# Linear attention and two mixtures of experts in one kernel: a unit's outputs placed beside the next unit's state products

## The reference

```
def _attn_ref(q, k, v, f_logit):
    f = 1.0 / (1.0 + np.exp(-f_logit))
    for t in range(S):
        state = f[:, :, t, :, None] * state + np.einsum('bhd,bhe->bhde', k[:, :, t], v[:, :, t])
        y[:, :, t] = np.einsum('bhd,bhde->bhe', q[:, :, t], state)

def _moe_ref(x, domain_probs, w1, w2):
    p = domain_probs / (domain_probs.sum(-1, keepdims=True) + 1e-09)
    for e in range(E):
        out += p[:, e:e + 1] * (np.maximum(x @ w1[e], 0.0) @ w2[e])
```

## Time and profile before

| | us |
|---|---|
| median of 3 runs (1073.31 to 1074.09) | 1073.92 |
| the profiled execution | 1075.53 |
| its span in the trace | 1073.8 |
| TensorE busy in the span | 1029.2 |
| units 5 to 31 with the first expert's pieces, about | 56.5 to 345 |

### The profile page before, as it was taken

How to read it: one execution, slowest core, us unless ns; L and a number is a source line. 1 busy time by engine, 2 the same in 40 slices (tenths; PEclk the granted TensorE clock), 3 DMA queues, 4 the chain that set the end, 5 groups by cost and what they waited for, 6 DMA issues and landing times.

```text
span 1073.8 us, 17708 instructions
## 1 busy us (share of the span) xinstructions
PE 1029.2 (96%) x6997; PEld 966.1 (90%) x6997; DVE 358.6 (33%) x773; ACT 279.9 (26%) x577; POOL 88.4 (8%) x109
## 2 busy tenths in 40 slices
PE   5799999999999999999999999999999999999895
PEld 5688888888899899999999999999999999999543
DVE  4545454554644222222222222222222222222323
ACT  3343233232332331111114111111322222222322
POOL 1340100001000230000005000000220000000000
PEclk9699999999999999999999999999999999999897
DMA  9522343323420330000000300000030004020684
GB/s 218 115 61 57 73 80 66 61 57 75 83 56 13 124 118 1 0 0 0 0 1 1 117 0 0 0 0 0 0 118 1 1 1 176 0 79 1 240 328 176
DMA packets 129761, 67.04 MB, mean 62 GB/s; under 512 B 106656, under 2 KB 125088, under 8 KB 129696
## 3 DMA queue, kind: packets, MB, share of 16 engines
q1 hardware_dynamic: 129696, 66.18, 22.3%
HBM read 56.72 MB, written 4.72 MB: 57 GB/s over the span
## 4 chain that ended last, share of the span: by engine, by line
PE 93%; DVE 2%; SPq 2%; issue 1%; DMA 0%; ACT 0%; DVEq 0%; ACTq 0%
PE ph L1242 13%; PE po L1261 12%; PE po L1259 12%; PE ph L1244 12%; PE po L1260 12%; PE ph L1243 12%; PE pair L1194 2%; PE pc L1218 2%; PE pair L1162 2%; PE pc L1223 2%; PE pair L1174 1%; PE ph L1391 1%; PE po L1406 1%; PE pair L1164 1%; PE pc L1202 1%
## 5 line engine op out<-in xcount | busy, mean ns | idle before, releaser
L969 DVE SCALAR_TENSOR_TENSOR h_lo<-ph,h_hi 128x384 fp32r<-128x384 f32 x256 | 142.6, 557 | 503.4 <-ACT h_hi L736 502.7
L736 ACT ACTIVATE h_hi<-ph 128x384 fp32r<-128x384 f32 x256 | 126.0, 492 | 563.6 <-PE ph L1244 563.6
L1242 PE MATMUL ph<-xT,w_hi 128*128 128x384 f32 (+1 forms) x768 | 266.4, 347 | 2.2 <-DVE xT L950 2.2
L1259 PE MATMUL po<-w_hi,h_hi 128*128 128x384 f32 x768 | 259.3, 338 | 0.0
L1244 PE MATMUL ph<-xT,w_lo 128*128 128x384 f32 (+1 forms) x768 | 257.3, 335 | 0.0
L1261 PE MATMUL po<-w_hi,h_lo 128*128 128x384 f32 x768 | 257.1, 335 | 0.0
L1243 PE MATMUL ph<-xT,w_hi 128*128 128x384 f32 (+1 forms) x768 | 256.9, 335 | 0.0
L1260 PE MATMUL po<-w_lo,h_hi 128*128 128x384 f32 x768 | 256.7, 334 | 0.0
L1242 PEld LDWEIGHTS ph<-xT,w_hi 128*128 128x128 f32 x768 | 144.2, 188 | 8.8 <-issue 4.7
L1243 PEld LDWEIGHTS ph<-xT,w_hi 128*128 128x128 f32 x768 | 144.4, 188 | 0.0
L1259 PEld LDWEIGHTS po<-w_hi,h_hi 128*128 128x128 f32 x768 | 144.2, 188 | 0.2
(11 more groups left out here) (169 smaller groups left out, 711.2 us busy)
## 6 DMA issues: line engine op xcount, KB each, us to landing
v<-in_moe_w_dram SPq DMA_DIRECT2D x15, 1536.0 KB, 10.7
raw<-in_moe_w_dram SPq DMA_DIRECT2D x8, 1536.0 KB, 8.8
f_in<-in_f_logit_dram SPq DMA_DIRECT2D x48, 96.0 KB, 2.6
k_in<-in_k_dram SPq DMA_DIRECT2D x48, 96.0 KB, 2.6
q_in<-in_q_dram SPq DMA_DIRECT2D x48, 96.0 KB, 2.6
v_in<-in_v_dram SPq DMA_DIRECT2D x48, 96.0 KB, 2.6
out_dram<-out_sb SPq DMA_DIRECT2D x5, 768.0 KB, 5.5
x_raw<-yT SPq DMA_DIRECT2D x48, 72.0 KB, 2.2
```

The source lines that it names most:

```text
L736: a.activation(h_hi[:, f % 2, :], ph[f % 2][:, 0:BLK], ACT.Relu).then_inc(h_hi_done, 1)
L969: d.scalar_tensor_tensor(out=h_lo[:, f % 2, :], in0=ph[f % 2][:, 0:BLK], scalar=0.0, in1=h_hi[:, f % 2, :].bitcast(F32), op0=ALU.max, op1= ...
L1242: t.matmul(bank, wh, xh, start=(kk == 0), stop=False, skip_group_check=True)
L1259: t.matmul(bank, hh, w2_hi[:, f, :], start=(f == 0), stop=False, skip_group_check=True)
```

## The change

There are four parts.

1. The products of a unit become a step of their own, `P`, after `S`. They go into spare columns of the same pair banks as the scores (384 to 479 of the first bank, 384 to 431 of the second). DVE now waits for the products before it masks, and in the same place for the outputs of the unit before.
2. `Y` of unit u moves behind `P` of unit u + 1, except for the last unit of a half (u % 4 == 3), whose Y keeps its place two pieces after P.
3. The running sums of C and D go to `pc` in place of `pair`, and C or D moves behind the unit's fourth piece, so that it stands directly ahead of the next unit's T.
4. Waits follow: C and D wait for the copied outputs and for the sums before them, Y for the sums taken from `pc`, T for the state additions of the unit before. `qT` alternates between two tiles.

```diff
@@ first_stage
         steps.append(("S", u, None))
+        steps.append(("P", u, None))
+        if u > LAG and u % PER_HALF:
+            steps.append(("Y", u - 1, None))
...
         steps.append(pieces[n + 2])
-        steps.append(("Y", u, None))
+        if u % PER_HALF == PER_HALF - 1:
+            steps.append(("Y", u, None))
+        steps.append(pieces[n + 3])
         if m + 1 < UNITS // 2:
             steps.append(("D" if u % 2 else "C", m + 1, None))
-        steps.append(pieces[n + 3])
...
+        def products_of(u, c):
+
+            at_col = BLK + (c if c < BT - 1 else 0) * D
+            return pair_of(u)[:, 0 if c < BT - 1 else 1, at_col:at_col + D]
+
         def sums_bank(m, part):
-            return ph[part] if m <= 2 else bT
+            return ph[part] if m <= 2 else bST
+
+        def before_y(u):
+
+            return 0 if u < LAG else min(u + (2 if u % PER_HALF == PER_HALF - 1 else 3), 2 * QUADS)
...
             def scores(u):
...
-                dve.wait_ge(s_filled, u + 1)
+                dve.wait_ge(p_filled, u + 1)
+                at_least(dve, y_filled, before(u) + 1)
...
-                dve.wait_ge(p_filled, u + 1)
-                bank = last_of(u)
...
-                        new = bank[rows, c * D:(c + 1) * D]
+                        new = products_of(u, c)[rows, :]
...
                 if m <= 2:
                     at_least(pe, c_taken, 2 * (m - 1) + part + 1)
                 else:
-                    pe.wait_ge(s_masked, 2 * (m - 1) + part + 1)
+                    u = 2 * (m - 1) + part
+                    pe.wait_ge(y_taken, u + 1 if u < LAG or u % PER_HALF == PER_HALF - 1 else u)
+                    pe.wait_ge(c_taken, 2 * m + part)
...
                 at_least(pe, s_masked, before(u) + 1)
+                at_least(pe, st_done, st_count(before(u) + 1))
...
-                if m >= 2:
-                    pe.wait_ge(c_taken, 2 * m + i + 2 if m + 1 < QUADS else 2 * QUADS)
...
-                mm.then_inc(s_filled, 1)
-                bank = last_of(u)
-                at_least(pe, y_taken, before(u) + 1)
+
+            def products(u):
+                m, i = divmod(u, 2)
                 pe.wait_ge(v_landed[m % 2], loaded(m))
...
                 pe.wait_ge(s_masked, u + 1)
                 pe.wait_ge(st_done, st_count(u + 1))
+                at_least(pe, y_taken, before(u) + 1)
+                at_least(pe, c_taken, before_y(u))
```

More of the change, by code:

```diff
@@ L27 @@
 OPENING = (
-    "G0 L0 C0 D0 G1 L1 T0 T1 C1 D1 S0 S1 Y0 Y1 T2 T3 G2 L2 S2 S3 C2 D2 Y2 Y3 "
-    "W0 W1 T4 G3 S4 L3 X0 W2 Y4 C3"
+    "G0 L0 C0 D0 G1 L1 T0 T1 C1 D1 S0 P0 S1 P1 Y0 Y1 T2 T3 G2 L2 S2 P2 S3 P3 C2 D2 Y2 Y3 "
+    "W0 W1 T4 G3 S4 P4 L3 X0 W2 Y4 C3"
 )
@@ L186, in build @@
     kT = [small("kT0", [P, BLK]), small_at(second, "kT1", [P, BLK])]
-    qT = [small("qT0", [P, BLK]), small_at(second, "qT1", [P, BLK])]
+    qT = [small(f"qT{i}", [P, BLK]) for i in range(2)]
     masked = [small("masked0", [P, 2, BT, P]), small_at(second, "masked1", [P, 2, BT, P])]
@@ L281, in build @@
         qT_done = sem("qT_done")
-        s_filled = sem("s_filled")
         p_filled = sem("p_filled")
@@ L701, in turn @@
                 act.wait_ge(q_turned, u + 1)
-                a.activation(qT[set_of(u)][:], pair_of(u)[:, 1, 0:BLK], ACT.Copy).then_inc(qT_done, 1)
+                a.activation(qT[u % 2][:], pair_of(u)[:, 1, 0:BLK], ACT.Copy).then_inc(qT_done, 1)
             def outputs(u):
@@ L1193, in scores @@
                         rows = slice(WIN * hh, WIN * (hh + 1))
-                        mm = t.matmul(banks[:, hh, cols], kT[s][rows, cols], qT[s][rows, cols], start=True, stop=True)
-                mm.then_inc(s_filled, 1)
-                bank = last_of(u)
-                at_least(pe, y_taken, before(u) + 1)
+                        mm = t.matmul(banks[:, hh, cols], kT[s][rows, cols], qT[u % 2][rows, cols], start=True, stop=True)
+            def products(u):
+                m, i = divmod(u, 2)
                 pe.wait_ge(v_landed[m % 2], loaded(m))
@@ L1201, in scores @@
                         head = 2 * i + hh
-                        mm = t.matmul(bank[WIN * hh:WIN * (hh + 1), c * D:(c + 1) * D], kd[m % 2][:, c, head, :],
+                        mm = t.matmul(products_of(u, c)[WIN * hh:WIN * (hh + 1), :], kd[m % 2][:, c, head, :],
                                       v_in[m % 2][:, c, head * D:(head + 1) * D], start=True, stop=True)
@@ L1222, in outputs @@
                             state = st[s][:, c - 1, hh, :] if c else carry[:, r, hh, :]
-                            mm = t.matmul(bank[WIN * hh:WIN * hh + D, cols], state, qT[s][:, cols],
+                            mm = t.matmul(bank[WIN * hh:WIN * hh + D, cols], state, qT[u % 2][:, cols],
                                           start=False, stop=True, skip_group_check=True)
@@ L1253, in sums @@
                     pe.wait_ge(y_taken, 4)
+                    pe.wait_ge(st_done, st_count(4))
                 if f == 0:
@@ L1273, in _ @@
                     scores(i)
+                elif kind == "P":
+                    products(i)
                 elif kind == "Y":
```

## The result

The changed kernel takes 1136.31 us (median of 4 runs, 1135.97 to 1136.37) against 1074.01 before: 1.0577 times as long, 95% interval 1.0563 to 1.0590. That is 62.3 us more. The forecast was 1128, with a range of 1102 to 1150.

A forecast was written before the change was run, and what follows sets the result against it. PE was taken to bound units 5 to 31, busy 284.30 of 288.50 us. The terms 20.3 + 20.4 + 3 - 4 + 2.2 + 12 = 53.9 on 1073.92 gave 1128 us, range 1102 to 1150.

The forecast's parts named there:

- Part 1: T directly behind D in odd units: the 2.83 us chain uncovered, 1.56 us at each of 13 places, +20.3 us.
- Part 2: k and q loaded late for C's multiplies, so S waits about 3.4 us at six places: +20.4 us.
- Part 3: DVE's queue at the units with X (8, 12, ... 28): C's multiplies enter the gap, 0.5 us each, +3 us.
- Part 4: Y joined to P and C to T: two fewer small/large matmul edges in about 20 units, -4 us.
- Part 5: Opening: C of quad 3 waits for unit 4's copied outputs, and DVE masks later; +2.2 us, from 0 to 4.
- Part 6: TensorE's clock falls behind 7 of 19 gaps, 1.7 us lost each: +12 us, from 0 to 32.
- the likeliest case: Both waits come and the clock falls at some gaps: 1128 us, 1120 to 1138, chance 0.5.
- The rival of full clock: Both waits come in units 5 to 31 but the clock stays up: 1116 us, chance 0.2.
- the one with loads in time: k and q arrive in time for C's multiplies, so Part 2 and its falls go: 1100 us, chance 0.12.
- The rival in which nearly every gap pays: The clock falls at nearly every gap ahead of T and S: 1148 us, chance 0.13.

The follow-up runs named there:

- filled gaps: Changed kernel with PE's idle time ahead of T of even units and S of units 7, 11, ... 27 filled by matmuls whose result is overwritten: 1113.8 us.
- the outputs in their place: Changed kernel, but Y of every unit stands two pieces behind its own S and P, as before the change: 1100.0 us.
- the first four edits: Edits of the changed kernel: C and D ahead of the fourth piece (1115.4 us), loads ahead of stores (1102.4), both (1076.6), idle time filled with matmuls (1113.8).
- the early loads: Changed kernel, but for units 5, 9, ... 25 SP issues gate, k and q loads ahead of the wait for the unit's copied outputs: 1102.4 us.
- the sums a piece earlier: Changed kernel, but C and D stand ahead of the unit's fourth piece again, so a piece lies between D and T: 1115.4 us.

## Why the prediction was right, point by point

The terms are set against units 5 to 31, from the starts of PE's instructions. The kernel with filled gaps serves as the changed kernel without the clock.

| part | forecast | measured |
|---|---|---|
| 1, T behind D | +20.3 | +21.2 |
| 2, late k and q | +20.4 | +23.6 |
| 3, DVE's queue at X | +3 | +0.4 |
| 4, joined edges | -4 | -7.8 |
| 5, opening | +2.2 | -0.3 |
| 6, clock | +12 | +24.2 |

**Part 1** held as it was worked out. The idle time at T is 25.3 us, and 4.1 of it were there before, so 21.2 are new. The number of places (13) and the chain's length (2.83, then 2.79) were both read rightly, and moving D back took T's waits away.

**Part 2** had the right place, number and cause. Each of the six costs 3.9 us rather than 3.4. In the one shown, the loads of k took 2.18 us on SP and not 1.54 as before; what held them the profile does not say.

**Part 3** was too high. With the loads late, X did not become the last to finish; the six S concerned start 0.42 us after the piece ahead, before 0.35.

**Part 4** was undersized by half. I counted two edges of 0.1 us; the rows of the changed kernel at P of unit 13 and Y of unit 12 show where the rest was:

```profile
164.34 0.44 PE L1215 MATMUL pair<-v_in,kd 128*64 128x48 f32 x8
164.60 0.39 PE L1233 MATMUL pc<-masked,v_in 128*48 128x128 f32 x4
164.82 0.39 PE L1238 MATMUL pc<-qT,carry 128*48 128x128 f32 x4
```

P to Y is 0.26 us, where P to the piece h was 0.37; and where two blocks of small matmuls become one, a slow first step of h and a way into Y go as well. I put that at 0.38 us a unit in 19 units, an estimate. The measured figure is a remainder of the account, 288.3 + 21.2 + 23.6 + 0.4 - 325.7 = 7.8, so it holds whatever else the order changed; the estimate from the outputs in their place (7 us, above) agrees.

**Part 5** did not show in this kernel. The wait was there, 1.9 us ahead of C of quad 3. What gave as much back was the clock: the long low stretch of the opening ends at 51.1 us here and at 53.5 before. C and the T behind it, from the start of C to the first full piece, take 2.0 us instead of 4.2. C and the piece in the changed kernel, then the piece before:

```profile
52.38 0.59 PE L1176 MATMUL pc<-f_in,causal 128*128 128x192 f32 x2 [1.88 <-ACT yT L721]
54.35 0.42 PE L1257 MATMUL ph<-xT,w_hi 128*128 128x384 f32 x1
```

```profile
54.70 0.42 PE L1242 MATMUL ph<-xT,w_hi 128*128 128x384 f32 x1
```

The forecast of the opening had no term for the clock. With its low stretch the opening varies more than the term: S of unit 5 starts between 56.2 and 59.7 us in the five profiles of kernels that have the changed opening and differ only later (the changed kernel and the first four edits), and at 55.5 to 56.5 in three with the old one. The low stretch is 13.7 us long in two of the five, where S starts at 56.2, and 17.1 or 20.5 in the others; it is 13.7 in the three. So what the change itself costs there stays open.

**Part 6** was the largest miss, half of its value: 24.2 us instead of 12. I had taken 7 falls of 3.4 us each. The trace of the changed kernel has 11 low stretches in the units with 58 us in all. Which gaps bring it down was read rightly, few of the 13 and most of the six: it was five of the 13, 3.4 us each, and all six, 6.8 us each. Both the number and the length were too low. The length was taken from one low stretch near the end of the kernel, though the opening, where it also fell, has longer ones (6.8 us from 22.7 us on, 13.7 from 39.8). Half of 58 us would be 29; that 24.2 were lost fits low time that lies in the gaps, as the first microsecond of the stretch from 191 does. By number of falls the forecast lay between its two rivals.

So the likeliest case came true, 8 us low, and the misses of parts 3 to 5 (-9) hid part of those of 2 and 6 (+15). The rival of full clock (1116) was refuted by 20 us, the one with loads in time (1100) by 36. The rival in which nearly every gap pays (1148) was 12 us off, and the eight gaps of T without a fall speak against it. The Trainium skill ("TensorE: Matmul & The Clock Gate", HAM oscillation) describes a loop that is granted the low clock anew in every round, and its waits there are longer than the 13 gaps of 2 us here. The trace agrees with it for the six long gaps, and for five of the 13 short ones.

## What to carry to other kernels

Count the distance from an instruction to the one that needs its result in time, not in steps: a step that looked free to move was the whole cover of a 2.8 us chain. When a result is moved later, read what is queued behind the wait for it on every queue; here twelve loads on SP held X up for 3 us, and passing the finished half on before them gave 5 us (1072.3 to 1066.9) to a kernel without the change. And price a gap with its clock: here 50 us of waits brought 24 us more.

## What had not been expected of the hardware

**Equal gaps, unequal clock.** Gaps of 2 us ahead of T, with the same work next to them, had a fall behind 5 of 13 in the changed kernel, 8 of 13 with the early loads and 1 of 13 with the outputs back, in one profile of each. The last two had PE busy for 288 and 286 us in the units. The gaps of 3.2 to 5.4 us ahead of S had one each time, six of six in the changed kernel and six of six with the sums a piece earlier. So the length of a gap of 2 us alone does not decide it. What else does, perhaps when it comes, was not tried.

**The clock at the end.** The part after the units is the same program in all of these kernels, and in the profiled executions took 727.5 to 734.0 us. The longest had the low clock for 30 us of the last 70, the shortest for 20; PE is not busy throughout there. So a difference of 2 or 3 us in the total of two such kernels need not come from the edit; the units' own length, read from the trace, is the better witness there.
